# An attention, routing and expert kernel: each K and V row loaded once, gate logits kept in PSUM, weight preparation moved, loops unrolled

## The reference, cut to what matters

```python
# B, H, S, D = 4, 8, 768, 64; n_mem = 8
for c in range(S // 32):
    q_c = q[:, :, c*32:c*32 + 32]
    k_full = concat([mem_k, k[:, :, max(0, c*32 - 16):min(S, c*32 + 40)]], axis=2)
    v_full = concat([mem_v, v[:, :, the same rows]], axis=2)
    a = softmax(q_c @ k_full.T / 8)
    out[:, :, c*32:c*32 + 32] = a @ v_full
x = out as [3072 tokens, 512]
```

## Time and profile before

| | us |
|---|---|
| median of three executions | 851.69 |
| the profiled execution | 851.32 |
| its span, first to last instruction | 849.3 |
| PE busy, share of the span | 716.4 (84%) |
| VectorE busy | 548.7 (65%) |
| ScalarE busy | 316.8 (37%) |
| GpSimd busy | 336.0 (40%) |

### The profile page before, as it was taken

One profiled execution on the slowest core, in us unless ns is written; L12 is line 12 of the kernel. 1 busy time (PEld: TensorE's weight loads), 2 busy tenths in 40 slices (PEclk: granted clock), 3 DMA queues, 4 the chain that ended last, 5 costly groups with the idle time before them and its releaser, 6 DMA issues.

```text
span 849.3 us, 17717 instructions
## 1 busy us (share of the span) xinstructions
PE 716.4 (84%) x6837; PEld 620.9 (73%) x6838; DVE 548.7 (65%) x2135; ACT 316.8 (37%) x521; POOL 336.0 (40%) x243
## 2 busy tenths in 40 slices
PE   4668768212998899989999998999899999989993
PEld 3546645101996888889888988888798889888982
DVE  3435535676869677967778696879677776832140
ACT  2223424002314631561355146315613551463170
POOL 6790000008515730771275157307713751572001
PEclk9879979655999999999999999999999999999997
DMA  8988963005103301330231033113302310331000
GB/s 347 350 290 287 398 216 106 10 0 185 51 1 112 113 37 51 100 99 25 79 119 53 26 112 114 49 51 100 100 26 83 114 52 26 112 121 42 1 12 37
DMA packets 24940, 89.33 MB, mean 105 GB/s; under 512 B 3360, under 2 KB 3360, under 8 KB 24864
## 3 DMA queue, kind: packets, MB, share of 16 engines
q0 software_dynamic: 14208, 50.34, 17.9%
q1 hardware_dynamic: 10656, 37.97, 12.4%
HBM read 75.71 MB, written 12.58 MB: 104 GB/s over the span
## 4 chain that ended last, share of the span: by engine, by line
PE 72%; issue 8%; DMA 6%; DVE 5%; POOL 5%; ACT 2%; SPq 0%; POOLq 0%; DVEq 0%; ACTq 0%
PE bank L503 19%; PE bank L505 18%; PE bank L504 18%; DMA raw<-w,w_idx 4%; PE bank L436 3%; POOL wl L1292 3%; PE bank L393 3%; PE banks L418 2%; PE bank L403 2%; PE bank L429 2%; PE banks L532 1%; DVE hits L958 1%; DVE hot_a L958 1%; DVE mask L958 1%; PE bank L532 1%
## 5 line engine op out<-in xcount | busy, mean ns | idle before, releaser
L1286 POOL DMA_INDIRECT raw<-w,w_idx x60 | 66.0, 1101 | 283.4 <-DVE w_idx L1007 246.1
L1292 POOL TENSOR_TENSOR wl<-raw,wh 128x1024 fp32r<-128x1024 f32 x60 | 149.5, 2492 | 21.3 <-ACT wh L729 20.3
L729 ACT ACTIVATE wh<-raw 128x1024 fp32r<-128x1024 f32 x60 | 63.4, 1056 | 100.5 <-DMA raw<-w,w_idx 100.5
L503 PE MATMUL bank<-xh,wh 128*128 128x384 f32 x256 | 92.7, 362 | 3.7 <-POOL wl L1292 3.3
L503 PE MATMUL bank<-hh,wh 128*128 128x384 f32 x256 | 90.1, 352 | 0.0
L505 PE MATMUL bank<-xh,wl 128*128 128x384 f32 x256 | 88.6, 346 | 0.0
L504 PE MATMUL bank<-xl,wh 128*128 128x384 f32 x256 | 88.5, 346 | 0.0
L505 PE MATMUL bank<-hh,wl 128*128 128x384 f32 x256 | 86.0, 336 | 0.0
L504 PE MATMUL bank<-hl,wh 128*128 128x384 f32 x256 | 85.9, 336 | 0.0
L503 PE MATMUL bank<-wout_h,uh 128*128 128x512 f32 x192 | 79.8, 415 | 0.1
L503 PE MATMUL bank<-win_h,yh 128*128 128x512 f32 x192 | 77.3, 403 | 0.0
(11 more groups left out here) (178 smaller groups left out, 1642.8 us busy)
## 6 DMA issues: line engine op xcount, KB each, us to landing
unit<-unit_in SPq DMA_DIRECT2D x24, 768.0 KB, 6.2
unit<-unit_in SPq DMA_DIRECT2D x24, 520.0 KB, 5.4
x_rows<-x_sb SPq DMA_DIRECT2D x24, 256.0 KB, 4.8
raw<-w_in POOLq DMA_DIRECT2D x4, 512.0 KB, 8.1
raw<-w_out POOLq DMA_DIRECT2D x4, 512.0 KB, 6.5
raw<-w,w_idx POOLq DMA_INDIRECT x60, 4.4
gath<-x_rows,ids POOLq DMA_INDIRECT x24, 3.5
out<-z,ids_prev POOLq DMA_INDIRECT x14, 2.8
```

Source lines behind the costliest of these rows:

```text
L503: nc.tensor.matmul(bank, stat_h, mov_h, start=first, stop=False)
L729: nc.scalar.activation(wh[:, c % WCH, :], stage(s, c), ACT.Copy).then_inc(w_hi, 1)
L1286: gp.indirect_dma_start(stage(s, c), None, table, bass.IndirectOffsetOnAxis(ap=w_idx[:, c % WCH:c % WCH + 1], axis=0))\
L1292: gp.tensor_tensor(wl[:, c % WCH, :], stage(s, c), wh[:, c % WCH, :].bitcast(F32), ALU.subtract)\
```

## The change

**Loads.** A unit's k is now one row of 152 keys (`SPAN`) with the 8 memory keys behind it, instead of four windows of 64 keys. The chunks read overlapping slices of it. V comes as 32 rows for each chunk and half of the partitions; the other 24 rows of a window are the first 24 rows of the next chunk's block. They are copied from partitions 0 to 23 of each half to partitions 32 to 55 by VectorE for one half and by ScalarE for the other (`next_front`), in a ring of 12 slots (`vr`). The memory rows of V are loaded into partitions 56 to 63 of each half for the first three units of each batch. A last small load brings the block behind the last unit.

**PE.** The scores are 32 products of 56 columns and 8 of 8 columns (all 128 queries of the unit against the memory keys). The gate has x as the stationary operand and writes token x expert logits straight into columns of PSUM that stay untouched until the end; VectorE reads them from there by two copies. The 24 transposes and ScalarE's copies to `logT` are gone.

**Order.** GpSimd's preparation waits until all loads of attention have landed. All loops of the attention are unrolled.

```diff
-QW, KW, VW = HP * P, HP * CPT * WIN, HP * CPT * (D + 1)
+KEYS = WIN - MEM
+SPAN = P + LEFT + RIGHT
+FRONT = LEFT + RIGHT
+QW, KW, VW = HP * P, HP * (SPAN + MEM), CPT * HP * (D + 1)
+RING = 3 * CPT
...
+        def next_front(engine, copy, a, u):
+            if u == 0:
+                engine.wait_ge(v_loaded[0], v_count(0))
+            engine.wait_ge(v_loaded[(u + 1) % 3], v_count(u + 1))
+            if u >= 3:
+                engine.wait_ge(pv_ps, u - 2)
+            own, after = slice(64 * a, 64 * a + FRONT), slice(64 * a + CHUNK, 64 * a + CHUNK + FRONT)
+            s = CPT * (u % 3)
+            if s + CPT < RING:
+                last = copy(vr[after, s:s + CPT, :, :], vr[own, s + 1:s + CPT + 1, :, :])
+            else:
+                copy(vr[after, s:RING - 1, :, :], vr[own, s + 1:RING, :, :])
+                last = copy(vr[after, RING - 1, :, :], vr[own, 0, :, :])
+            last.then_inc(v_next[a], 1)
...
+            def load_v(u):
+                if u >= 3:
                     sp.wait_ge(pv_ps, u - 2)
+                slots = slice(CPT * (u % 3), CPT * (u % 3) + (CPT if u < NT else 1))
+                for a in range(2):
+                    if u % TPB < 3 and u < NT:
+                        sp.dma_start(vr[64 * a + 64 - MEM:64 * a + 64, slots, :, :].rearrange("p c h d -> p (c h d)"),
+                                     v_mem[u // TPB, a, :, :]).then_inc(v_loaded[u % 3], 16)
+                    own = vr[64 * a:64 * a + CHUNK, slots, :, :].rearrange("p c h d -> p (c h d)")
+                    sp.dma_start(own, v_in[u, a, :, 0:own.shape[1]]).then_inc(v_loaded[u % 3], 16)
...
+            for u in range(NT):
+                if u + 4 < NT:
+                    load_qk(u + 4)
+                if u + 3 <= NT:
+                    load_v(u + 3)
                 store(u, u)
...
-                                S_PS[r % 2][a][CHUNK * c:CHUNK * (c + 1), hp * WIN:(hp + 1) * WIN],
-                                q[rows, hp, CHUNK * c:CHUNK * (c + 1)], k[rows, hp, c, :], start=True, stop=True)
+                                S_PS[r % 2][a][CHUNK * c:CHUNK * (c + 1), hp * WIN:hp * WIN + KEYS],
+                                q[rows, hp, CHUNK * c:CHUNK * (c + 1)], k[rows, hp, CHUNK * c:CHUNK * c + KEYS],
+                                start=True, stop=True)
+                for hp in range(HP):
+                    for a in range(2):
+                        rows = slice(64 * a, 64 * a + 64)
+                        mm = nc.tensor.matmul(S_PS[r % 2][a][:, hp * WIN + KEYS:(hp + 1) * WIN],
+                                              q[rows, hp, :], k[rows, hp, SPAN:SPAN + MEM], start=True, stop=True)
...
-                    mm = nc.tensor.matmul(GATE_PS[r % 2], wg[:, k, :], xT[:, r % 2, k, :], start=(k == 0), stop=(k == KD - 1))
+                    mm = nc.tensor.matmul(LOGITS[u % 2][:, u // 2 * E:(u // 2 + 1) * E], xT[:, r % 2, k, :], wg[:, k, :],
+                                          start=(k == 0), stop=(k == KD - 1))
...
-            with pe.Fori(1, B) as b:
-                for r in range(TPB):
-                    step(b * TPB + r, r, b * 2 + (r // 3 + 1), b * 2 + ((r - 1) // 3 + 1))
...
-            pe.wait_ge(gate_sb, NT)
-            for t in range(NT):
-                mm = nc.tensor.transpose(PS[0][:, t * E:(t + 1) * E], logT[:, t * P:(t + 1) * P], ident[0:E, 0:E])
-            mm.then_inc(logits_ps, 1)
...
+                    next_front(act, lambda to, of: nc.scalar.activation(to, of, ACT.Copy), 1, i)
...
+                next_front(ve, lambda to, of: nc.vector.tensor_copy(to, of), 0, u)
...
+            ve.wait_ge(gate_ps, NT)
+            for i in range(2):
+                last = nc.vector.tensor_copy(M[:, :, :, :].rearrange("p j e (t i) -> p j e t i", i=2)[:, :, :, :, i],
+                                             LOGITS[i].rearrange("p (j t e) -> p j e t", j=2, t=TG // 2))
...
             gp.wait_ge(small_in, 32)
+            for i in range(3):
+                gp.wait_ge(qk_loaded[i], 16 * (NT // 3))
+            gp.wait_ge(v_loaded[0], v_count(NT))
             prep_load(0)
```

More of the change, by code:

```diff
@@ L191, in build @@
         gate_ps = sem("gate_ps")
-        gate_sb = sem("gate_sb")
-        logits_ps = sem("logits_ps")
+        v_next = [sem(f"v_next{a}") for a in range(2)]
         dve = sem("dve")
@@ L289, in build @@
         q_of = lambda i: unit[:, i, 0:QW].rearrange("p (h q) -> p h q", h=HP)
[L290 to L291 removed]
+        k_of = lambda i: unit[:, i, QW:QW + KW].rearrange("p (h w) -> p h w", h=HP)
         S_PS = [[PS[0], PS[1]], [PS[2], PS[3]]]
         PT_PS, XT_PS = PS[6], PS[7]
[L295 removed]
+        LOGITS = [S_PS[i][0][:, HP * WIN:HP * WIN + NT // 2 * E] for i in range(2)]
         MM = [PS[0], PS[1], PS[2]]
@@ L339, in _, with load_qk @@
             sp.dma_start(gain[:, :], g_ln).then_inc(small_in, 16)
-            def load_qk(u, r, first=False):
-                if not first:
+            def load_qk(u):
+                if u >= 3:
                     sp.wait_ge(scores_ps, u - 2)
[L344 to L348, removed]
+                sp.dma_start(unit[:, u % 3, :], qk_in[u, :, :]).then_inc(qk_loaded[u % 3], 16)
@@ L353, in store @@
             def store(u, r):
                 sp.wait_ge(x_ready, u + 1)
-                sp.dma_start(x_dram[bass.ds(u * P, P), :], x_sb[:, r % 3, :, :, :].rearrange("p a b d -> p (a b d)"))\
+                sp.dma_start(x_dram[u * P:u * P + P, :], x_sb[:, r % 3, :, :, :].rearrange("p a b d -> p (a b d)"))\
                   .then_inc(x_stored[r % 3], 16)
[L358 to L366, removed]
-                for r in range(TPB):
[L368 to L372, removed]
+            load_qk(0)
+            load_qk(1)
+            load_v(0)
@@ L379, in _, with scores @@
         def _(pe):
[L380 to L383, removed]
+            def scores(u, r):
+                pe.wait_ge(qk_loaded[r % 3], 16 * (u // 3 + 1))
+                if u >= 2:
                     pe.wait_ge(shifted, u - 1)
-                if not (isinstance(u, int) and u < 4):
-                    pe.wait_ge(gate_sb, u - 3)
                 pe.sem_inc(pe_past, 1)
@@ L405, in probs_T, with values @@
                 mm.then_inc(pT_ps, 1)
-            def values(u, r, n):
+            def values(u, r):
                 pe.wait_ge(pT_sb, u + 1)
-                pe.wait_ge(v_loaded[r % 3], 16 * n)
-                if not (isinstance(u, int) and u < 1):
+                for a in range(2):
+                    pe.wait_ge(v_next[a], u + 1)
+                if u >= 1:
                     pe.wait_ge(x_ready, u)
                 pe.sem_inc(pe_past, 1)
-                v = v_of(r % 3)
                 for hp in range(HP):
@@ L435, in gate @@
                 for k in range(KD):
[L436 removed]
+                    mm = nc.tensor.matmul(LOGITS[u % 2][:, u // 2 * E:(u // 2 + 1) * E], xT[:, r % 2, k, :], wg[:, k, :],
+                                          start=(k == 0), stop=(k == KD - 1))
                 mm.then_inc(gate_ps, 1)
[L439 to L451, removed]
             pe.wait_ge(consts, 1)
             pe.wait_ge(small_in, 32)
[L455 to L467 removed]
+            for i in range(NT + 3):
+                if i < NT:
+                    scores(i, i % TPB)
+                if 1 <= i <= NT:
+                    probs_T(i - 1, (i - 1) % TPB)
+                if i >= 3:
+                    gate(i - 3, (i - 3) % TPB)
+                if 2 <= i <= NT + 1:
+                    x_T(i - 2, (i - 2) % TPB)
+                if 1 <= i <= NT:
+                    values(i - 1, (i - 1) % TPB)
             def best_T(f):
```

113 lines of the change are left out of this document (54 added, 59 removed).

## The result

The changed kernel takes 882.98 us (median of 4 runs, 877.46 to 883.52), the one before 850.32 beside it (847.99 to 852.1). The ratio is 1.037, with a 95% interval of 1.032 to 1.042: slower by 3.7%, where 852 was forecast and 869 was the upper end of the range. The profiled execution of the changed kernel has a span of 881.8 us, that of the one before 849.3.

A forecast was written before the change was run, and what follows sets the result against it. Attention was taken as bound by PE's instruction fetch, in pages of 126 matmuls. Routing start 13.4 + 131.1 + 7.7 = 152.2 us (-0.3) and preparation +0.5 gave 851.5, as a median 852 us; range 835 to 869.

The forecast's parts named there:

- the middle term: Attention after the second instruction block: 27.9 blocks of 126 matmuls, paced by fetching at 4.7 us each, 131.1 us.
- The second page: Start of attention: PE gets its second block of instructions, after 221 matmuls, at 13.4 us instead of 16.42.
- The 27.9 pages: Attention's 3519 matmuls in instruction blocks of 126, at 4.7 us each (ends 4.1 and 5.3): 131.1 us.
- The last steps: End of attention: from the last scores through the last gate and two copies to the routing, 7.7 us.
- 152.2: Forecast start of the routing in us, 13.4 + 131.1 + 7.7, against 152.47 before: 0.3 us less.
- The page theory: Attention: PE stands still when its next block of 126 matmuls' instructions has not come; 4.7 us a block.
- Rival (b): Attention: instruction fetching is hidden, PE alone needs 3.3 us per block of 126 matmuls, 813 us; chance 0.08.
- Rival (a): Attention: instruction blocks come faster, 4.1 to 4.5 us, with smaller load bursts; 841 us at 4.3; chance 0.26.
- Rival (c): Attention: instruction blocks stay at 5.0 to 5.3 us, fetches waiting behind load batches; 860 to 869 us; chance 0.24.
- New waits on V: Attention: VectorE and ScalarE wait for the next unit's V before copying; taken as nothing, bounds -0 and +10 us.
- rival (d): Slower by new waits: V late for its copies, or GpSimd's preparation late by up to 5 us; 856 to 862; chance 0.08.
- The preparation's +0.5 us: GpSimd's preparation, moved behind attention's loads, meets the gather's indices; 0.5 us added, bounds 0 and 5 us.

## Why the prediction was wrong

- **The step that failed** is the middle term's "That is 4.17 us, or 3.3 us a page. ... The page's fetch is longer." All three prices in it were read from rows at full clock, and their upper bound, 5.2 us a unit, from the gate's 1.04 us at full clock too. At 1.2 GHz a unit is 7.24 us and a page 5.7, above the whole range of 4.1 to 5.3. The earlier trace rows has clocks of 0.89, 1.00, 0.81 and 0.89 for the same engine, and I passed over that column. The mistake is not one of size: the bound changed from the fetch to PE itself, at a speed that the code of before had only for a unit or two at a time, behind a stop.
- **The terms, side by side.** The second page comes at 14.98 us, as forecast after 221 matmuls (13.4; 1.6 late). The 27.9 pages take 159.6 us, 5.72 each (131.1 at 4.7; +28.5). The last steps take 10.7 us (7.7; +3.0), since they too run at 1.2 GHz. That is 33.1 us above 152.2, which is 185.3 as measured.
- **The clock as the cause** is shown by the pair of the changed kernel and the one with both products widened: 883 against 856 us with no work removed. Widening the gate alone gives 16 of the 26.6 us (866.9), the memory products alone none (886.0). The low clock costs this much only because PE has 160 matmuls a unit: with 144, at 0.63 to 0.70, the time is 857.79. Which property of the mix decides, and why the changed kernel was granted its full clock again up to 76 us and not after it, stays open.
- **A rule that would have led the other way.** PE is busy for 22.25 of 23 us at 0.50. The Trainium skill (TensorE: Matmul & The Clock Gate, What's actually happening) says that the clock follows how busy PE has been recently, and releases with activity. Read by the busy share of the profile, it would give the higher level here and about 852 us; the measurement decides against that reading.
- **The page theory held,** where PE isn't the bound. The forecast of 4.7 us a page, for this very traffic, is 4.69 in the kernel with both products widened, and the kernel with a short loop body has hardly a stop and is 17 us faster than the kernel before. That 4.69 hits so closely is in part luck: the same working gives 4.9 us for the kernel with both PE changes undone (221 GB/s, 1.16 MB a page), which has 5.23, and 5.27 was measured at 292 GB/s. The page's price does not simply follow the bytes. Rival (b) was right about the trace, few stops, for a reason that it did not name; its 813 us would have needed the fetch to be hidden at full clock. The Trainium skill (Runtime: NRT & Kernel Launch, Instruction fetch mechanics) prefers unrolling, and here the kernel with the loop is 2.4% faster (835.23 for 856.0, the same work written out with three buffers): the measurement goes the other way.
- **Rival (a)** had pages of 4.1 to 4.5 us from smaller bursts; 4.69 at the same traffic speaks against it. **Rival (c)** lost its price to the same cause: its 5.0 to 5.3 us would have been right for the kernel with both PE changes undone (5.23).
- **New waits on V: none to speak of in the changed kernel, as forecast.** VectorE waited once, 0.6 us, and ScalarE once, 0.9 us, for V; VectorE's copies take 0.69 us in the middle. That holds because PE is slow: in the short loop ScalarE waits 15.4 us for V. Of rival (d), the late preparation fell as well: 7.09 us in hand.
- **The preparation's +0.5 us** can't be told from the nothing that three pairs of kernels show (852.99 beside 853.63, 836.59 for 835.23, 856.35 for 856.43), and it is luck, since the kind was wrong. I asked only whether GpSimd would be late. The price, 1.9 us between the routing's start and the gather in the changed kernel, is on VectorE, whose mask and value steps take 0.95 and 1.58 us instead of 0.36 each; in the pairs about as much is won in attention.
- **The median of 856.4 for the kernel with both products widened** is 4.4 above my 852. Its pages are as forecast; the second comes at 18.05 us for 13.4 and the 17 small operations keep VectorE 3.4 us past the last gate. Neither was in the sum.

## What to carry to other kernels

Price a change to PE's instruction mix at both clocks, and read the clock's column before trusting any duration: in this kernel products of 8 columns behind a full weight load cost the clock for everything around them, and padding them with zeros was faster. Where code is straight and PE stops in the middle of groups with no semaphore, shorten what it must fetch: the kernel with a short loop body gained 17 us here, and the bytes saved gained nothing. Before moving work to an idle stretch of one engine, look at what the other engines do there, not only at whether that engine will be in time.

## What the hardware showed that I had not expected

- PE stayed at 0.50 from about 77 us to the end of attention, some 107 us, while busy for 97% of the two stretches shown; more columns in 24 of its 160 matmuls a unit brought it to 0.94 to 1.00 from 79 to 150 us.
- PE's loop of about 1,190 instructions ran its later passes with stops of at most 0.5 us, one at each jump back; that of about 1,780 (before) ran one pass free, behind a stop of 0.49 us at the jump, and stood still for 7.3 us at the jump into the next. In the kernel with the preparation held back this repeats:

```profile
97.48 0.86 PE L418 MATMUL banks<-unit,pT 64*32 64x65 f32 x64
105.98 1.17 PE L393 MATMUL bank<-unit 64*32 64x64 f32 x64 [7.63 <-issue]
```

  Why the second pass is free and the third isn't remains open.
- Beside GpSimd's elementwise work, VectorE's operation on two tensors went from 0.36 to 0.95 and 1.58 us, and 17 small operations with one input tensor from 1.29 us to as much as 7.57 (with the gate of before and K loaded once), while L944, also with one input, kept its 0.48. In the kernel with both products widened it hits another step: the operation that scales the mask, with one input, takes 2.28 us for 0.26, and ends at 162.72 us, 0.12 us after the GpSimd subtraction that runs from 160.26 to 162.60; the value step behind it has its 0.36 again.

```profile
160.44 2.28 DVE L950 TENSOR_SCALAR mask<-mask 128x192 f32<-128x192 f32 x1
```

  The Trainium skill (GPSIMD Engine Reference, 1. Specifications) names contention for the shared SBUF interfaces with VectorE's instructions that have two SBUF inputs or run in a two-port mode. The 0.95 and 1.58 agree; whether the 17 and the 2.28 are of such a mode no run here shows.
